# Order of record fetches, weight splits and bounds around the last token tile and the first two expert tiles

## The chip, the cores and the metric

The kernel runs on one core of one Trainium2 chip. The metric is the time on the device in microseconds (us), the median of several executions. A core has a matrix engine (TensorE, "PE" in the profile, its weight loads "PEld"), VectorE ("DVE"), ScalarE ("ACT"), GpSimd ("POOL") and a sync engine ("SP") that only issues DMAs. Each engine runs its own program in order; semaphores are the only ties between them.

## The reference

Three steps, all in float32:

1. Attention within chunks of 64 rows, 8 batches, 8 heads, 576 rows, head size 64: softmax(q k^T / 8) v. The result is reshaped to 4608 tokens of 512 values.
2. A dense layer: h = x w_in (512 to 2048), r = max(h, 0), g = s r^2 + b, x2 = g w_out (2048 to 512).
3. A mixture of 8 experts with a skip: out starts as a copy of x2. For each token with x2 . w_skip > 0, the expert e is the argmax of x2 w_gate, its weight is the softmax value of that expert, and out = x2 + weight * (max(x2 w1[e], 0) w2[e]), with w1[e] 512 x 1024 and w2[e] 1024 x 512. Other tokens keep x2.

## The kernel before, in words

Every product is made of three: each operand is split into a high part (fp32r, made by ScalarE) and a low part (the rest, made by VectorE), and lo\*hi, hi\*lo and hi\*hi are summed in PSUM. So every weight and every activation has two "split" instructions, first on ScalarE, then on VectorE, which waits for it.

**Stage 1** goes over 12 tiles of 384 tokens. Within a tile a loop over f = 0..15 (FT = 16 blocks of 128 of the 2048 columns) makes h block f + 1 (`into_h`), and adds block f to x2 (`into_x2`); ScalarE makes relu, square and the high part of g (`relu`, `hi_of_g`), VectorE the low part (`lo_of_g`). Attention for the next tile is made between them. Tile 11 is the last and has no attention beside it; its spare time on ScalarE and VectorE is used to split the weights of experts 0 and 1. These come in 8 pieces of 512 KB each (EXPERT_JOBS = 8), numbered (e,j). `jobs_at(f)` says which pieces are split in step f (of expert 0 in the odd steps from 3 on, of expert 1 from SOON_AT = 9 on, up to piece 6 of both); both engines call `split2` for them at the end of the step. The sync engine loads the next piece into a buffer when the piece before it in the same buffer has been split (`soon_done[e]`).

**Routing.** For each tile x2 is kept (`keep_x2`), multiplied by the gate, and `route_a`, `rank` (on TensorE) and `route_b` find for each token a slot in a table of records (token number, weight) in DRAM, sorted by expert. GpSimd writes the records of a tile with three scatters (`send_records`). VectorE's last steps after tile 11 count the expert tiles: the chain of small instructions L1372 to L1385 writes `bounds`, which all engines read into registers before their loops over the experts.

**Stage 2** goes over expert tiles k of 128 records, each of one expert. Tiles 0 and 1 are the first tiles of experts 0 and 1 and hold records of the first eleven token tiles only, so that they can start before tile 11 is routed; tile 2 and all later ones need all records. For tile k: the sync engine fetches 128 records into `got` (`load_records`); VectorE copies them to `idx` (`next_records`); GpSimd gathers the rows of x2 (`gather`, into `x_rows`); TensorE turns them (`turn_rows`); ScalarE and VectorE split them (`hi_of_x`, `lo_of_x`); TensorE makes h in two halves of 512 columns (`up`), ScalarE the relu (`relu2`), TensorE turns h (`turn_h`), the halves are split (`hi_of_h`, `lo_of_h`), and `down` makes y, which `finish` weighs and adds to the row; a scatter writes it to out. In TensorE's program for tile k (`expert_tile`) the order is: turn h half 0 of k, up half 1 of k, turn the rows of k + 1, down with half 0 of k, turn h half 1 of k, up half 0 of k + 1, down with half 1 of k.

Between the stages TensorE turns the rows of tile 0, turns x2 of tile 11 (L875), and multiplies it by the gate (L881) from `tail_x`, which ScalarE copies out of PSUM. The sync engine's program runs there, in this order: the weight loads by `jobs_at`, the fetch of records 0 (after the jobs of f = 11) and 1, loads of expert 2's pieces 2, 0 and 3, the stores of tile 11's x2, pieces 7 and 1, pieces 4 to 6, then the wait for `bounds`, and the fetches of records 2 and on. Pieces 0 to 3 and 7 of expert 2 use the buffers in which the last pieces of experts 0 and 1 lie until they are split: buffer 0 holds (1,6), 1 holds (1,7), 2 holds (1,5), 3 holds (0,6), 7 holds (0,7).

Of the kernel before, what the change touches and what calls it, by code (L numbers as in the profile page):

```python
# [17 lines left out]
def chunked_attention_moe(nc, first_qk_rows, first_v_rows, qk, v, w_in, w_out, moe_s, moe_b, gate_rows, gate_cols_in, w1, w2, out):  # L18
# [6 lines left out]
    FT = FF // P  # L25
# [46 lines left out]
    with ctx:  # L72
# [266 lines left out]
        def raw_place(e, j):  # L339

            if soon(e):
                return raw2[((3, 7)[j % 2], j % 3)[e]]
            return raw2[j]

        def jobs_at(f):

            found = []
            if f % 2 == 1 and f >= 3:
                found.append((0, (f - 3) // 2))
            if f >= SOON_AT:  # L350
                found.append((1, f - SOON_AT))
            return found
# [17 lines left out]
        def _(sp):  # L370
# [96 lines left out]
            for j in range(3):  # L467
                load_weights(sp, 1, j)
            for f in range(3, FT - 2):
                for e, j in jobs_at(f):  # L470
                    sp.wait_ge(soon_done[e], j + 1)
                    load_weights(sp, e, j + (2, 3)[e])
                if f == FT - 5:
                    sp.wait_ge(records_out, 16 * SUB * (TILES - 1))
                    load_records(0, 0)
            load_records(1, REGION)
            for e, n in ((1, 2), (1, 0), (0, 3)):
                last = max(j for j in range(EXPERT_JOBS - 1) if raw_place(e, j) is raw2[n])
                sp.wait_ge(soon_done[e], last + 1)
                load_weights(sp, SOON, n)  # L480
            store_rows(TILES - 1)
            for e, n in ((0, 7), (1, 1)):
                sp.wait_ge(soon_done[e], EXPERT_JOBS)
                load_weights(sp, SOON, n)
            sp.wait_ge(x2_stored, 32 * TILES)
# [8 lines left out]
            with sp.Fori(2, first_end) as t:  # L494
                load_records(t, t * P - P)
            with sp.Fori(0, second_end - first_end) as t:
                load_records(first_end + t, REGION + P + t * P)
# [413 lines left out]
        def _(act):  # L911
# [159 lines left out]

            hi_of_x(0)
            for t in range(SUB):
                act.wait_ge(tail_turned, t + 1)
                keep(tail_x[:, t, :, :], y_ps[t][:, :]).then_inc(tail_kept, 1)
            split2(0, 1, EXPERT_JOBS - 1)
            split2(1, 0, EXPERT_JOBS - 1)
            route_exp(TILES - 1)
            relu2(0, 0)
            expert_tile(0, 0, 1, False, False)  # L1080
            expert_tile(1, 1, 0, False, False)
# [20 lines left out]
        def _(dve):  # L1102
# [141 lines left out]
            def tile(i, z, attend, route):  # L1244
                for f in range(FT):
# [27 lines left out]
                    for e, j in jobs_at(f) if not attend else ():  # L1273
                        split2(e, 1 - e, j)
                    if not attend and f == FT - 2:
                        dve.wait_ge(got_in, 16)
                        dve.tensor_copy(idx[:, :], got[:, :]).then_inc(rows_held, 16)
# [83 lines left out]
            dve.tensor_copy(sent[:, :], held[:, :]).then_inc(y_ready, 32)  # L1361
            split2(0, 1, EXPERT_JOBS - 1)
            dve.wait_ge(tail_done, 1)
            dve.tensor_copy(logits[:, :, :].rearrange("p t e -> p (t e)"), logits_ps).then_inc(dots_done, DOTS)
            route_a(TILES - 1)
            route_b(TILES - 1)

            def step(n, ins):
# [16 lines left out]
            dve.tensor_copy(bounds[:, :], bounds_f[:, :]).then_inc(bounds_ready, 1)  # L1385
            lo_of_h(0, 0)
            lo_of_x(1)
            stage_rows(1)
            lo_of_h(0, 1)
            split2(1, 0, EXPERT_JOBS - 1)  # L1390
            dve.wait_ge(next_ready, 1)
            next_records(2)
            finish(0)
            take_rows(1)
# [77 lines left out]
```

## Time and profile before

| | us |
|---|---|
| median of 3 runs | 1361.82 |
| lowest, highest | 1359.89, 1362.25 |
| the profiled execution | 1362.1 |
| its span, first to last instruction | 1360.3 |
| TensorE busy | 1327.8 (98%) |
| VectorE busy | 925.6 (68%) |
| ScalarE busy | 752.6 (55%) |
| GpSimd busy | 310.3 (23%) |
| mean granted clock of TensorE | 0.994 |

How to read the rows further down. Times are us from the start of the span. A row of a timeline has the start, the duration, the engine, the line of the kernel, the operation, output <- inputs, their shapes, how often it is repeated, and in brackets how long the engine was idle before it and what ended that. A row of the windows has the stretch and its length, then busy time and number of instructions of TensorE, its weight loads, VectorE, ScalarE and GpSimd, then TensorE's granted clock as a share of 2.4 GHz, the busy share of the DMA engines, and GB/s. A row of waits has who waited, for whom, the total in us, how many times, and the longest. "to landing" is the time from the issue of a DMA to its completion, as minimum, median and maximum over the DMAs of the view. In the chain of waits each row is a step of the chain: start, length, what.

### The profile page before, as it was taken

To read this page: it belongs to the slowest core of one execution; us is meant where nothing else is said; L and a number is where in the kernel's file an instruction comes from. 1 tells how busy PE (TensorE), PEld (TensorE's weight loads), DVE (VectorE), ACT (ScalarE), POOL (GpSimd) and SP (SyncE) were. 2 spreads that over 40 slices of the span, in tenths; PEclk is the share of its full clock that TensorE was granted. 3 is DMA by queue.
4 is the path that set the end of the run, shared out by engine and by line. 5 is a ranking of instruction groups with operands and counts; after the bars stand their busy time and mean duration, and the time that the engine had idled before them with its cause. 6 is when DMAs were issued, how large, how long until landed. Compare 5 with 4: busy or idle time off the path is not lost.

```text
span 1360.3 us, 22394 instructions
## 1 busy us (share of the span) xinstructions
PE 1327.8 (98%) x7066; PEld 1169.1 (86%) x7067; DVE 925.6 (68%) x2141; ACT 752.6 (55%) x1838; POOL 310.3 (23%) x274
## 2 busy tenths in 40 slices
PE   8999999999999999999999999999898999999998
PEld 7998989899998999899998999988676778888886
DVE  4877879687886978778786878876538673333332
ACT  4886757476665656566575666646337552222221
POOL 5542222121213222221322222101111111111111
PEclk9999999999999999999999999999999999999999
DMA  7431203031221303021120302045518641111110
GB/s 276 163 121 44 98 28 108 16 100 35 72 65 34 105 21 105 25 78 59 43 94 25 102 24 101 13 155 143 189 38 293 229 156 46 39 46 39 46 38 27
DMA packets 61589, 116.95 MB, mean 86 GB/s; under 512 B 11848, under 2 KB 20296, under 8 KB 61360
## 3 DMA queue, kind: packets, MB, share of 16 engines
q1 hardware_dynamic: 44496, 81.11, 18.1%
q10 hardware_dynamic: 10880, 20.97, 4.3%
q0 software_dynamic: 6112, 13.56, 3.0%
q8 instruction: 58, 0.95, 0.3%
q14 instruction: 43, 0.35, 0.1%
HBM read 91.28 MB, written 27.08 MB: 87 GB/s over the span
## 4 chain that ended last, share of the span: by engine, by line
PE 89%; DVE 4%; issue 3%; DMA 2%; SPq 1%; DVEq 1%; ACT 1%; POOLq 0%; ACTq 0%
PE h_ps L720 30%; PE y_ps L735 28%; PE y_ps L845 10%; PE h_ps L831 10%; PE s_ps L685 3%; PE av_ps L701 3%; DVE weights_lo L1171 2%; PE t_ps L692 1%; PE t_ps L817 1%; PE s_ps L839 1%; PE av_ps L839 1%; DMA first_raw<-in_first_qk 1%; DMA wide<-x_rows,idx 1%; DVE rows_t_lo L1304 0%; DVE wide L1337 0%
## 5 line engine op out<-in xcount | busy, mean ns | idle before, releaser
L1198 DVE CUSTOM_DVE_ANT_0 products<-scratch,wide 128x512 f32<-128x512 f32 x297 | 285.6, 962 | 6.7
L720 PE MATMUL h_ps<-rows_t_hi,weights_lo 128*128 128x384 f32 (+2 forms) x776 | 262.3, 338 | 8.0 <-issue 5.8
L720 PE MATMUL h_ps<-rows_t_hi,weights_hi 128*128 128x384 f32 (+2 forms) x776 | 261.3, 337 | 0.0
L720 PE MATMUL h_ps<-rows_t_lo,weights_hi 128*128 128x384 f32 (+2 forms) x776 | 260.0, 335 | 0.0
L982 ACT ACTIVATE scratch<-h_ps 128x384 f32<-128x384 f32 x192 | 94.4, 492 | 297.0 <-PE h_ps L720 294.9
L735 PE MATMUL y_ps<-weights_hi,g_lo 128*128 128x512 f32 x576 | 229.3, 398 | 1.5 <-DVE g_lo L1177 1.5
L735 PE MATMUL y_ps<-weights_lo,g_hi 128*128 128x512 f32 x576 | 227.4, 395 | 0.0
L735 PE MATMUL y_ps<-weights_hi,g_hi 128*128 128x512 f32 x576 | 226.7, 393 | 0.0
L1177 DVE TENSOR_TENSOR g_lo<-scratch,g_hi 128x384 fp32r<-128x384 f32 x192 | 119.9, 625 | 92.1 <-ACT g_hi L913 89.5
L720 PEld LDWEIGHTS h_ps<-rows_t_hi,weights_lo 128*128 128x128 f32 x776 | 145.9, 188 | 21.7 <-issue 7.5
L541 POOL TENSOR_TENSOR qk_lo<-qk_raw,qk_hi 128x768 fp32r<-128x768 f32 x66 | 124.7, 1890 | 144.8 <-ACT qk_hi L913 144.8
L720 PEld LDWEIGHTS h_ps<-rows_t_lo,weights_hi 128*128 128x128 f32 x776 | 145.9, 188 | 7.0
L547 POOL TENSOR_TENSOR v_lo<-v_raw,v_hi 128x256 fp32r<-128x256 f32 x66 | 49.1, 745 | 436.9 <-ACT v_hi L913 436.9
L720 PEld LDWEIGHTS h_ps<-rows_t_hi,weights_hi 128*128 128x128 f32 x776 | 145.8, 188 | 0.0
L735 PEld LDWEIGHTS y_ps<-weights_hi,g_hi 128*128 128x128 f32 x576 | 108.7, 189 | 24.0
L735 PEld LDWEIGHTS y_ps<-weights_hi,g_lo 128*128 128x128 f32 x576 | 108.9, 189 | 20.7 <-DVE g_lo L1177 2.8
L735 PEld LDWEIGHTS y_ps<-weights_lo,g_hi 128*128 128x128 f32 x576 | 108.9, 189 | 17.1 <-issue 0.2
L930 ACT ACTIVATE soft<-s_ps,row_bias 64x64 f32<-64x64 f32 x528 | 120.2, 303 | 3.0
L913 ACT ACTIVATE rows_t_hi<-av_ps 64x256 fp32r<-64x256 f32 (+2 forms) x165 | 67.9, 412 | 69.9 <-PE av_ps L839 64.3
L913 ACT ACTIVATE g_hi<-scratch 128x384 fp32r<-128x384 f32 x192 | 100.8, 525 | 6.1
L845 PE MATMUL y_ps<-weights_hi,rows_t_lo 128*128 128x512 f32 x240 | 97.7, 407 | 6.5 <-DVE rows_t_lo L1304 5.5
L986 ACT ACTIVATE scratch<-scratch 128x384 f32<-128x384 f32 x192 | 99.7, 519 | 3.5
(178 smaller groups left out, 2366.3 us busy)
## 6 DMA issues: line engine op xcount, KB each, us to landing
qk_raw<-in_qk SPq DMA_DIRECT2D x66, 384.0 KB, 2.9
expert_raw<-in_w ACTq DMA_DIRECT2D x25, 512.0 KB, 5.1
expert_raw<-in_w SPq DMA_DIRECT2D x21, 512.0 KB, 5.3
out<-scratch SPq DMA_DIRECT2D x12, 768.0 KB, 4.2
x_rows<-scratch SPq DMA_DIRECT2D x12, 768.0 KB, 6.0
v_raw<-in_v SPq DMA_DIRECT2D x66, 128.0 KB, 2.0
scratch<-in_w ACTq DMA_DIRECT2D x15, 512.0 KB, 5.9
wide<-in_w_out SPq DMA_DIRECT2D x7, 512.0 KB, 4.4
```

The source lines that it names most:

```text
L541: pool.tensor_tensor(qk_rest[:, :], qk_raw[:, c % SLOTS, :], qk_top[:, :].bitcast(F32), ALU.subtract).then_inc(qk_split, 1)
L547: pool.tensor_tensor(v_lo[:, :], v_raw[:, :], v_hi[:, :].bitcast(F32), ALU.subtract).then_inc(v_split, 1)
L720: mm = pe.matmul(h_ps[f % 2][:, begin:end], w[:, f // PAIR, kt, fs], x[:, z, kt, begin:end], start=kt == 0 and n == 0, stop=kt == KT - 1 a ...
L735: mm = pe.matmul(y_ps[t][:, :], g[:, f % 2, ts], w[:, f, :], start=f == 0 and n == 0, stop=f == FT - 1 and n == 2)
L831: mm = pe.matmul(h_ps[f][:, :], x[:, kt, :], w[par][:, f, kt, :], start=kt == 0 and n == 0, stop=kt == KT - 1 and n == 2)
L845: mm = pe.matmul(y_ps[0][:, :], h[:, t, :], w[par][:, t, :], start=t == 0 and n == 0, stop=t == ET - 1 and n == 2)
L913: return act.activation(out_, in_, ACT.Copy)
L930: last = act.activation(probs[xs, c % 2, h, :], s_blocks[xs, h, x, :], ACT.Exp, bias=row_bias[xs, h:h + 1], scale=SCALE)
L982: act.activation(r_buf[f % 2], h_ps[f % 2][:, 0:TOK], ACT.Relu).then_inc(r_done, 1)
L986: act.activation(u_buf[f % 2], r_buf[f % 2], ACT.Square).then_inc(u_done, 1)
L1177: dve.tensor_tensor(GL[:, f % 2, :], u_buf[f % 2], GH[:, f % 2, :].bitcast(F32), ALU.subtract).then_inc(g_ready, 1)
L1198: dve.tensor_tensor_reduce(products[:, :], x2_sb[:, t, :], gate_w[:, e, :], 1.0, 0.0, ALU.mult, ALU.add, logits[:, t, e:e + 1]).then_inc(d ...
```

## The change

No computation is added or removed; seven places in the programs of the sync engine, ScalarE and VectorE change their order.

- `jobs_at` no longer gives jobs for f = 15; pieces (0,6) and (1,6) are split after the tail tile.
- The sync engine waits for tile 10's scatters and fetches record set 0 ahead of the jobs of f = 10 instead of after those of f = 11; VectorE copies it to `idx` at the end of f = 12 instead of f = 14.
- The sync engine loads expert 2's piece 2, stores tile 11, loads pieces 3 and 7, then 4 to 6. Pieces 0 and 1 are loaded only after the fetch of the records of tile 2 (the loop from 2 to `first_end`, which has one pass in this trace).
- ScalarE splits (0,6) after turning tile 0's rows and ahead of copying `tail_x`, (0,7) after these copies, (1,6) after `hi_of_x(1)`, and (1,7) after `hi_of_h(0,1)`.
- VectorE splits (0,6) ahead of the wait for the logits, (0,7) between `route_a` and `route_b`, (1,6) after `stage_rows(1)`, and (1,7) after `next_records(2)`.
- VectorE's `lo_of_h(0, 0)` goes ahead of the bounds.

```diff
--- before.py
+++ after.py
@@ -345,9 +345,9 @@
         def jobs_at(f):
 
             found = []
-            if f % 2 == 1 and f >= 3:
+            if f % 2 == 1 and 3 <= f < FT - 1:
                 found.append((0, (f - 3) // 2))
-            if f >= SOON_AT:
+            if SOON_AT <= f < FT - 1:
                 found.append((1, f - SOON_AT))
             return found
 
@@ -467,21 +467,20 @@
             for j in range(3):
                 load_weights(sp, 1, j)
             for f in range(3, FT - 2):
+                if f == FT - 6:
+                    sp.wait_ge(records_out, 16 * SUB * (TILES - 1))
+                    load_records(0, 0)
                 for e, j in jobs_at(f):
                     sp.wait_ge(soon_done[e], j + 1)
                     load_weights(sp, e, j + (2, 3)[e])
-                if f == FT - 5:
-                    sp.wait_ge(records_out, 16 * SUB * (TILES - 1))
-                    load_records(0, 0)
             load_records(1, REGION)
-            for e, n in ((1, 2), (1, 0), (0, 3)):
-                last = max(j for j in range(EXPERT_JOBS - 1) if raw_place(e, j) is raw2[n])
-                sp.wait_ge(soon_done[e], last + 1)
-                load_weights(sp, SOON, n)
+            sp.wait_ge(soon_done[1], EXPERT_JOBS - 2)
+            load_weights(sp, SOON, 2)
             store_rows(TILES - 1)
-            for e, n in ((0, 7), (1, 1)):
-                sp.wait_ge(soon_done[e], EXPERT_JOBS)
-                load_weights(sp, SOON, n)
+            sp.wait_ge(soon_done[0], EXPERT_JOBS - 1)
+            load_weights(sp, SOON, 3)
+            sp.wait_ge(soon_done[0], EXPERT_JOBS)
+            load_weights(sp, SOON, 7)
             sp.wait_ge(x2_stored, 32 * TILES)
             sp.wait_ge(tail_done, 1)
             for j in range(4, EXPERT_JOBS - 1):
@@ -493,6 +492,10 @@
             sp.wait_ge(records_out, 16 * SUB * TILES)
             with sp.Fori(2, first_end) as t:
                 load_records(t, t * P - P)
+            sp.wait_ge(soon_done[1], EXPERT_JOBS - 1)
+            load_weights(sp, SOON, 0)
+            sp.wait_ge(soon_done[1], EXPERT_JOBS)
+            load_weights(sp, SOON, 1)
             with sp.Fori(0, second_end - first_end) as t:
                 load_records(first_end + t, REGION + P + t * P)
             with sp.Fori(2, E) as e:
@@ -1070,14 +1073,20 @@
                 load_weights(nc.scalar, e, j)
 
             hi_of_x(0)
+            split2(0, 1, EXPERT_JOBS - 2)
             for t in range(SUB):
                 act.wait_ge(tail_turned, t + 1)
                 keep(tail_x[:, t, :, :], y_ps[t][:, :]).then_inc(tail_kept, 1)
             split2(0, 1, EXPERT_JOBS - 1)
-            split2(1, 0, EXPERT_JOBS - 1)
             route_exp(TILES - 1)
             relu2(0, 0)
-            expert_tile(0, 0, 1, False, False)
+            hi_of_h(0, 0)
+            relu2(0, 1)
+            hi_of_x(1)
+            split2(1, 0, EXPERT_JOBS - 2)
+            hi_of_h(0, 1)
+            split2(1, 0, EXPERT_JOBS - 1)
+            relu2(1, 0)
             expert_tile(1, 1, 0, False, False)
             act.wait_ge(bounds_ready, 1)
 
@@ -1272,7 +1281,7 @@
                         split(EARLY + f)
                     for e, j in jobs_at(f) if not attend else ():
                         split2(e, 1 - e, j)
-                    if not attend and f == FT - 2:
+                    if not attend and f == FT - 4:
                         dve.wait_ge(got_in, 16)
                         dve.tensor_copy(idx[:, :], got[:, :]).then_inc(rows_held, 16)
 
@@ -1359,11 +1368,13 @@
             dve.wait_ge(rows_taken, 1)
             next_records(1)
             dve.tensor_copy(sent[:, :], held[:, :]).then_inc(y_ready, 32)
-            split2(0, 1, EXPERT_JOBS - 1)
+            split2(0, 1, EXPERT_JOBS - 2)
             dve.wait_ge(tail_done, 1)
             dve.tensor_copy(logits[:, :, :].rearrange("p t e -> p (t e)"), logits_ps).then_inc(dots_done, DOTS)
             route_a(TILES - 1)
+            split2(0, 1, EXPERT_JOBS - 1)
             route_b(TILES - 1)
+            lo_of_h(0, 0)
 
             def step(n, ins):
                 ins.then_inc(bounds_step, 1)
@@ -1383,13 +1394,13 @@
             step(9 + E, dve.tensor_scalar(bounds_f[:, E + 2:E + 3], bounds_f[:, E:E + 1], 16.0, 32.0, ALU.mult, ALU.add))
             step(10 + E, dve.tensor_scalar(bounds_f[:, E + 3:], bounds_f[:, 1:E + 1], -1.0, None, ALU.add))
             dve.tensor_copy(bounds[:, :], bounds_f[:, :]).then_inc(bounds_ready, 1)
-            lo_of_h(0, 0)
             lo_of_x(1)
             stage_rows(1)
+            split2(1, 0, EXPERT_JOBS - 2)
             lo_of_h(0, 1)
-            split2(1, 0, EXPERT_JOBS - 1)
             dve.wait_ge(next_ready, 1)
             next_records(2)
+            split2(1, 0, EXPERT_JOBS - 1)
             finish(0)
             take_rows(1)
             expert_tile(1, 1, 0, False)
```

## Rows read from the trace of the kernel before

**Rows 1.** Busy time by engine, granted clock and DMA, 20 us each (the windows).

```profile
980.00:1000.00 20.00, 13.46 (x58) 10.79 (x57) 4.13 (x12) 2.97 (x5) 3.08 (x3) 0.83 0.26 94
1000.00:1020.00 20.00, 19.79 (x98) 16.07 (x97) 9.60 (x21) 9.42 (x14) 3.04 (x3) 1.00 0.12 42
```

**Rows 2.** TensorE's timeline (start, duration, ..., [idle before <- releaser]), 978 to 1010 us.

```profile
982.33 0.39 PE L831 MATMUL h_ps<-weights_hi,rows_t_hi 128*128 128x512 f32 x1
989.25 1.09 PE L817 MATMUL t_ps<-ident,wide 128*128 128x128 f32 x4 [6.54 <-DMA wide<-x_rows,idx]
...
993.89 0.60 PE L839 MATMUL av_ps<-ident,wide 128*128 128x128 f32 x4
...
1003.01 0.60 PE L817 MATMUL t_ps<-ident,wide 128*128 128x128 f32 x4
...
1006.42 0.60 PE L839 MATMUL av_ps<-ident,wide 128*128 128x128 f32 x4
```

**Rows 3.** The chain of waits in order of time (start, length, what).

```profile
975.39 1.14 DVE weights_lo L1171
...
978.52 0.48 SPq L491
...
980.21 4.63 DMA got<-table
...
986.03 3.09 DMA wide<-x_rows,idx
```

**Rows 4.** The sync engine's own waits, 950 to 982 us.

```profile
SPq L364 <- DVE weights_lo L1171: 20.8, 3, 13.5
```

**Rows 5.** The three record scatters of tile 10: issue times, time to landing.

```profile
L560 POOL DMA_INDIRECT table<-record,slot x3: 972/1301/1843, 932.2 to 936.0; - x3
...
DMA to landing us min/median/max: 5.3/6.6/10.4
```

**Rows 6.** The three record scatters of tile 11: issue times, time to landing.

```profile
L560 POOL DMA_INDIRECT table<-record,slot x3: 973/992/1024, 966.9 to 969.5; - x3
...
DMA to landing us min/median/max: 3.4/3.5/3.7
```

**Rows 7.** Landing of the five expert-weight loads issued 933 to 940 us.

```profile
DMA to landing us min/median/max: 3.6/9.0/9.8
```

**Rows 8.** Landing of the four expert-weight loads issued 976 to 979 us.

```profile
DMA to landing us min/median/max: 3.7/5.4/6.7
```

**Rows 9.** Landing of the record fetches issued 940 to 1000 us.

```profile
DMA to landing us min/median/max: 1.7/2.7/4.6
```

**Rows 10.** Landing of the row gathers issued 900 to 1000 us.

```profile
DMA to landing us min/median/max: 2.5/4.0/7.0
```

**Rows 11.** ScalarE's timeline, 940 to 965 us.

```profile
945.05 1.99 ACT L913 ACTIVATE weights_hi<-expert_raw 128x1024 fp32r<-128x1024 f32 x2
947.73 0.49 ACT L982 ACTIVATE scratch<-h_ps 128x384 f32<-128x384 f32 x1 [0.68 <-PE h_ps L720]
...
958.85 1.57 ACT L913 ACTIVATE scratch<-y_ps 128x512 f32<-128x512 f32 x3
```

**Rows 12.** VectorE's timeline, 955 to 975 us.

```profile
956.78 2.06 DVE L1187 SCALAR_TENSOR_TENSOR scratch<-y_ps,s_col,bias 128x512 f32<-128x512 f32 x3
...
961.39 1.23 DVE L1171 TENSOR_TENSOR weights_lo<-expert_raw,weights_hi 128x1024 fp32r<-128x1024 f32 x1 [0.98 <-ACT weights_hi L913]
...
965.80 0.16 DVE L1240 TENSOR_TENSOR slot<-slot_f,far 128x3 int32<-128x3 f32 x1
...
969.82 0.67 DVE L1304 TENSOR_TENSOR rows_t_lo<-s_ps,rows_t_hi 128x512 fp32r<-128x512 f32 x1
```

**Rows 13.** TensorE's timeline, 955 to 975 us.

```profile
957.69 0.63 PE L817 MATMUL t_ps<-ident,wide 128*128 128x128 f32 x4 [1.17 <-DMA wide<-x_rows,idx]
...
959.58 2.82 PE L881 MATMUL s_ps<-gate_cols,scratch 128*128 128x9 f32 x24
...
970.59 0.47 PE L845 MATMUL y_ps<-weights_hi,rows_t_lo 128*128 128x512 f32 x1 [0.48 <-issue]
```

## The prediction, made before the changed kernel was run

> **What bounds the kernel now.** TensorE is busy nearly everywhere, so I looked for the stretch where it is not. The windows of 20 us come first: from 980 to 1000 us TensorE is busy for 13.46 us at a mean granted clock of 0.83, from 1000 to 1020 for 19.79 us at 1.00 [rows 1]. All that the change touches lies between 930 and 1010 us, so the second view is TensorE's timeline there. Its last product of expert tile 1's second half of h starts at 982.33; then it idles 6.54 us until the rows gathered for tile 2 have landed, at 989.25 [rows 2]. The next tile's copy of the same stretch (transposes of rows, twelve products, transposes of h) takes 1006.42 - 1003.01 = 3.41 us. The h products are spaced 0.23 us, so without the wait the transposes would start at 982.56 and the next ones at 985.97; they start at 993.89. The stall thus costs 7.92 us: 6.7 of waiting and the rest at the lower clock, since the granted clock is 0.83 on average in this window, that is, TensorE came out of its idleness at 1.2 GHz instead of 2.4 (its four transposes take 1.09 us beside 0.60 in the next tile [rows 2]).
>
> Third, the chain of waits tells what made the rows late [rows 3]: VectorE's last split of expert 1 (975.39), then the sync engine's loads, its register loads of the bounds from 978.52, the fetch of the records at 980.21, which takes 4.63 us, and the gather at 986.03, which takes 3.09. The sync engine stood 13.5 us on that split [rows 4] with load (1,1) of expert 2. Behind it in its program stood three more loads and the fetch of the records for tile 2, for which everything else was ready: the bounds were being finished when lo_of_h(0,0), the next VectorE instruction after them, began at 969.82 [rows 12], and the third scatter of tile 11's records, issued at 969.5, landed at 969.5 + 3.7 = 973.2 [rows 6]. So the fetch could have gone 7 us earlier.
>
> **Part 1, the fetch of tile 2's records (the main term).** Removed: the wait on split (1,7) ahead of the loads and of the fetch. Moved: loads 0 and 1 of expert 2 behind the fetch. I follow the new chain. Split (0,7) now sits between route_a and route_b. It costs 1.23 us on VectorE [rows 12], some 0.4 of which is won back because the logits are copied about 0.3 us earlier and nothing stands ahead of them. The slot of the records, at 965.80 before, comes at 966.63, 0.83 later, and the third scatter is issued at 970.3. lo_of_h(0,0) now stands ahead of the bounds (0.67 us, and about 0.4 of waiting for its high half), so the bounds, 969.9 before, are ready at 971.7. The sync engine's register loads take 980.21 - 978.52 = 1.7 us [rows 3], to 973.4; they do not bind, the scatter does. It lands at 973.8 to 974.0 if it takes 3.4 to 3.7 us as before [rows 6]. But four loads of 512 KB (pieces 7, 4, 5, 6), which in the kernel before are issued from 976.5 on, now go out at 965.2 to 966.7, ahead of and beside the scatters. Their old group needed up to 6.7 us each to land [rows 8], 8.2 us from first issue to last landing; from 965.2 that ends at 973.4. Bounds for the scatter: 3.4 us [rows 6], and 10.4 us, which the last scatter of tile 10 took among five such loads [rows 5, 7]. I take 4.2, nearer the quiet rows, since all four loads are out 3.6 us before this scatter, while tile 10's last had three issued after it and beside it: landed at 974.5. The fetch follows at 974.9 and lands after 1.7 us (bounds 1.7 and 4.6 [rows 9]; 4.6 was with four loads just ahead of it, now the queue is empty), at 976.7. Before, the gather started at 986.03, 1.2 us after the fetch had landed at 980.21 + 4.63 = 984.84 [rows 3], with the copy into idx between them; VectorE is free from 974.6 on, so the gather starts at 977.9. It needs 2.5 to 7.0 us [rows 10]; loads 0 and 1, 1 MB, now go out at 975.4 and 978.2 beside it, so I take 4.2, by the 4.0 of the middle row: 982.1.
>
> When does TensorE want it? Parts 2 and 3 bring it there 0.6 us earlier than 982.56, at 981.9. A wait of about 0.3 us stays, too short to lower the clock by anything seen here. Part 1: 7.92 - 0.3 = 7.6 us gained.
>
> The Trainium skill, page "DMA: Bandwidth & Descriptors", section "Queues, rings and completion order", says two things that pull apart here. Its arbitration rule lets each DMA engine take turns between queues packet by packet; by that the scatter would land in its quiet 3.5 us and the sum would be 0.3 us better. Its ordering rule says that the write which raises a semaphore lands only after every earlier write of that DMA engine, across its queues; by that rule the scatter's completion waits for the loads' data, as the 10.4 us row looks, and it speaks against putting four loads ahead of it: the sum would be as I have it or, with loads that drain slowly, that of rival A.
>
> **Part 2, what moves out of the tail (f = 15).** Splits (0,6) and (1,6) leave VectorE ahead of keep_x2. keep_x2 started at 956.78 only because two splits were in front [rows 12]; TensorE had ended its last product at 957.69 - 1.17 = 956.52 [rows 13], so the three parts can now follow the products as they end, and the last is kept some 1.4 us earlier. The 1.17 us of idleness ahead of turn_rows(0) ended with the gather of tile 0's rows [rows 13]; its records are now fetched before the loads of f = 10 and copied at f = 12, so these rows land several us earlier and this wait goes too. But what TensorE needs next is tail_x from ScalarE, whose three copies began at 958.85 [rows 11]. ScalarE now turns x at 957.2 and then has split (0,6), 1.0 us (two take 1.99 [rows 11]), ahead of these copies: they begin at 958.7. So of 1.2 us on TensorE only 0.15 reach the logits (959.58 before [rows 13]). Bounds: 0 and 1.2.
>
> **Part 3, lo_of_h(0,0) ahead of the bounds.** Before, VectorE did it at 969.82, behind the bounds, and TensorE's down products waited 0.48 us for it, to 970.59 [rows 12, 13]. It now runs at 967.5, and the wait goes: 0.48 gained. Late next is lo_of_x(1), behind the bounds: 971.7 to 972.4, wanted by first_half(1) at 973.15, so 0.7 us of cover is left; beyond it each us of bounds is a us of TensorE. Splits (1,6) and (1,7) fall into time in which VectorE had nothing to do between its split at 975.39 and the fetch's landing at 984.84 [rows 3], and (1,7), done by 978.1, is wanted only at 982.4. Expert 2's pieces 0 and 1 land by 983; ScalarE first reads them some 22 us later, so that costs nothing.
>
> **Part 4, the price in the tail tile.** At f = 10 the sync engine now waits for tile 10's scatters ahead of loads (1,4), (0,6), (1,5). The last scatter was issued at 936.0 and landed after 10.4 us, at 946.4 [rows 5], among these very loads, whose own landing took up to 9.8 us [rows 7]. With three of them held back I expect it to land at about 942 (bounds 939.4 by the quiet 3.4 us [rows 6], and 946.4). Load (1,4) goes out at 942.4 and lands by about 947 (3.7 to 5.4 us [rows 8]). ScalarE wants it at 946.0, the second of the pair at 945.05, and has 0.68 us to spare before the next relu [rows 11]; TensorE has a block of h products of about 2 us between that relu and its use. So nothing is lost until the load lands after about 948.3, that is, unless the scatter lands after 943.4. VectorE's new wait for the records, at f = 12, holds lo_of_g(13) behind it; it ends at 944 to 945, when that instruction is due anyway. I take 0.
>
> **Sum.** 7.6 + 0.15 + 0.48 = 8.2 us off the profiled execution's 1362.1 us (span 1360.3): 1353.9. That execution is 0.3 us above the median of the runs, 1361.82; I predict 1353.7 for the median.
>
> **Rivals.** A: the loads delay the records and something of the stall stays. The scatter takes 6.6 us [rows 5], to 976.9, fetch to 979.0, gather started 980.3, 4.0 us, landed 984.3: 2.4 us of wait, 1356.0. For it: rows 5 and 7. Against it: rows 8, where four loads drained in 8.2 us. B: the records of tile 10 still land at 946.4, so (1,4) lands at 946.8 + 3.7 = 950.5; ScalarE's split is 950.5 - 946.0 = 4.5 us late, 3.8 after its slack. TensorE loses between 0 and 3.8, I take the middle, 1.9: 1355.6. C: the wait changes its owner. Scatter and fetch both meet the loads at their worst, 10.4 and 4.6 us, and gather 5.0 beside loads 0 and 1: 970.3 + 10.4 + 0.4 + 4.6 + 1.2 + 5.0 = 991.9, later than 989.25 by 2.7 us, so the kernel is slower, 1364.5. It decides from the scatter's landing on: with these fetch and gather times the stall is as long as before when it takes 7.7 us, and it is longer beyond. D: the fetch lands no earlier than before because only part of this comes true (scatter 7.7 us): 1361.8 less the small gains, about 1361.
>
> **Numbers.** Forecast 0.61, A 0.17, B 0.13, C 0.04, D 0.05. The forecast's own range is 1352.4 (all 1.2 us of part 2, no wait left) to 1355.2. A and B, also together, reach to 1358, and I add 0.9 us below for the scatter of the runs: 1351.5 to 1358.2. A measurement of this kernel can tell 0.2%, 2.7 us, from no change. Forecast, A and B are faster by more; D is the same; C is at the edge. So 0.91, 0.05, 0.04.
>
> **What would show it.** Right: a fetch at about 975 us in the trace, no idleness over 1 us ahead of TensorE's transposes at 982, granted clock 1.00 from 980 to 1000, no 0.48 us ahead of the down products, and logits at about the old time. Wrong: a fetch later than 978 (A, C), ScalarE waiting for a weight load at 946 to 950 (B), TensorE waiting for lo_of_x(1), or a gather of 5 us or more.

## The result, and the profile after

The changed kernel takes 1352.53 us (median of 5 runs, 1352.33 to 1355.31) beside 1362.24 us of the kernel before: a ratio of 0.9938, 95% interval 0.9923 to 0.9954. That is 9.7 us less; the interval allows 6.3 to 10.5. The forecast was 1353.7 us, 8.2 us less than before. The two profiled executions, 1362.1 and 1355.16 us, lie 6.9 us apart: the one of the changed kernel is 2.6 us above its median.

The stall is gone. The windows of the changed kernel, beside [rows 1]:

```profile
980.00:1000.00 20.00, 20.00 (x101) 16.39 (x100) 7.10 (x18) 4.57 (x8) 3.25 (x4) 1.00 0.17 57
```

TensorE's timeline of the changed kernel answers to [rows 2, 13]; the numbers in front are start and duration:

```profile
958.41 3.79 PE L884 MATMUL s_ps<-gate_cols,scratch 128*128 128x9 f32 x24 [0.90 <-ACT scratch L916]
968.21 0.66 PE L842 MATMUL s_ps<-ident,wide 128*128 128x128 f32 x4 [0.69 <-ACT wide L1040]
971.46 0.60 PE L820 MATMUL t_ps<-ident,wide 128*128 128x128 f32 x4
974.65 0.60 PE L842 MATMUL av_ps<-ident,wide 128*128 128x128 f32 x4
983.77 0.60 PE L820 MATMUL t_ps<-ident,wide 128*128 128x128 f32 x4
986.98 0.60 PE L842 MATMUL av_ps<-ident,wide 128*128 128x128 f32 x4
```

No transposes of rows (L820) have a bracket: TensorE waits for no gather, neither at 955.60 nor at 983.77. But the logits take 3.79 us instead of 2.82, and this is the surprise of the trace. The windows of the changed kernel show why (the third column from the right is the granted clock):

```profile
955.00:960.00 5.00, 4.10 (x35) 3.71 (x33) 4.02 (x9) 3.76 (x6) 0.90 (x1) 1.00 0.51 190
960.00:966.00 6.00, 6.00 (x21) 4.84 (x20) 3.31 (x14) 0.41 (x2) 0.29 (x1) 0.50 0.72 237
```

From 960 to 966 us TensorE has work all the time and only the 1.2 GHz level of its clock. In the profiled execution of before this time was at full clock. The windows of the kernel before:

```profile
960.00:966.00 6.00, 5.57 (x43) 4.55 (x42) 4.42 (x23) 2.92 (x5) 1.00 (x1) 1.00 1.02 367
```

The sync engine's waits from 940 to 990 us, beside [rows 4]:

```profile
SPq L490 <- DVE bounds L1396: 6.4, 1, 6.4
...
SPq L493 <- DMA table<-record,slot: 0.3, 1, 0.3
```

It now waits for the bounds and then 0.3 us for the last scatter, and fetches at 975.66 what it fetched at 980.21; the copy into idx runs at 977.50:

```profile
977.50 0.17 DVE L1320 COPY idx<-got 128x2 int32<-128x2 int32 x1 [0.90 <-DMA got<-table]
```

**One measure for all traces.** Stage 1 ends anywhere within some 6 us from one execution to the next. So I compare a *stretch* within each trace: from the first product of the last tail block (it has the bracket "DVE g_lo") to the h transposes of tile 1 (av_ps, the second one). It begins here in TensorE's timelines, before and changed:

```profile
954.16 0.50 PE L735 MATMUL y_ps<-weights_hi,g_lo 128*128 128x512 f32 x1 [0.20 <-DVE g_lo L1177]
```

```profile
953.41 0.50 PE L738 MATMUL y_ps<-weights_hi,g_lo 128*128 128x512 f32 x1 [0.20 <-DVE g_lo L1186]
```

Before: 954.16 to 993.89, 39.73 us. Changed: 953.41 to 986.98, 33.57 us. What is left after it, 1360.3 - 993.89 and 1353.4 - 986.98, is 366.4 us in both. Ahead of it, the tail tile from its first x2 block (f = 0) to its last (f = 15) takes 61.8 us in all fourteen traces (61.77 to 61.85), with the change and without. What differs is the start of that tile, from 889.1 to 894.7 us, and no instruction ahead of it was changed. So in the traces all of the change's effect lies in the stretch. ScalarE's timeline of the changed kernel has the relu of [rows 11] with the same 0.68 us to spare:

```profile
946.98 0.49 ACT L985 ACTIVATE scratch<-h_ps 128x384 f32<-128x384 f32 x1 [0.68 <-PE h_ps L723]
```

Its 6.16 us come apart like this. The stall: by the changed kernel's own undisturbed tile (986.98 - 983.77 = 3.21 us) it had cost 993.89 - 982.56 - 3.21 = 8.12 us. From the last block to the logits 5.42 became 5.00: 0.42. From turn_rows(1) to the next transposes, 973.43 - 969.51 = 3.92 before [rows 13 hold the wait in it], 3.19 now: 0.73. The logits and the products after them, up to the h transposes (959.58 to 966.25 before, 6.67 us), take 968.21 - 958.41 = 9.80 us: 3.13 lost to the clock. Sum: 8.12 + 0.42 + 0.73 - 3.13 = 6.14. The medians differ by 9.7 us, 3.5 more than the stretch; no trace shows where, since the executions at the median were not profiled.

### The profile page after: what moved, and what is told of

Same layout as the page of the kernel before. It is cut to its first block, busy times and chain, and to the rows that moved or that the text cites. A ratio compares the mean times of both kernels' runs of the same rounds, so it can differ in the third digit from the quotient of the medians.

```text
span 1353.4 us, 22395 instructions
## 1 busy us (share of the span) xinstructions
PE 1329.0 (98%) x7066; PEld 1171.8 (87%) x7067; DVE 927.9 (69%) x2141; ACT 753.0 (56%) x1838; POOL 311.1 (23%) x274
## 4 chain that ended last, share of the span: by engine, by line
PE 90%; DVE 5%; issue 3%; ACT 1%; DVEq 1%; POOLq 0%; POOL 0%; ACTq 0%
PE h_ps L723 29%; PE y_ps L738 28%; PE y_ps L848 10%; PE h_ps L834 10%; PE s_ps L688 3%; PE av_ps L704 3%; DVE weights_lo L1180 2%; PE t_ps L695 1%; PE s_ps L842 1%; PE t_ps L820 1%; PE av_ps L842 1%; PE h_ps L651 0%; DVE rows_t_lo L1313 0%; DVE weights_lo L1171 0%; DVE g_lo L1186 0%
## 5 line engine op out<-in xcount | busy, mean ns | idle before, releaser
L834 PE MATMUL h_ps<-weights_hi,rows_t_lo 128*128 128x512 f32 x244 | 102.1, 418 | 0.0
```

The costliest lines, as they stand in the source:

```text
L834: mm = pe.matmul(h_ps[f][:, :], x[:, kt, :], w[par][:, f, kt, :], start=kt == 0 and n == 0, stop=kt == KT - 1 and n == 2)
```

## The experiments

The kernels ran in groups, each group on one chip with the kernel before beside it, whose medians were 1363.20 us (e1 to e4), 1363.06 (e5, e7, e8, e9), 1366.17 (e6, e10, e11) and 1362.66 (e12). Between groups the ratio and the stretch can be compared, the bare times cannot. The ratios of the kernels other than e2 and e10 have intervals that overlap: the runs' times alone separate none of them, and what follows rests on the traces, one of each kernel.

| kernel | median us | ratio, 95% | stretch us | low clock in 955 to 970 | wait for gather 2 |
|---|---|---|---|---|---|
| before | 1362.24 | | 39.73 | none | 6.54 |
| changed | 1352.53 | 0.9938 (0.9923 to 0.9954) | 33.57 | long | none |
| e9, changed again | 1353.11 | 0.9928 (0.9912 to 0.9944) | 33.55 | long | none |
| e11, changed again | 1356.93 (one run) | | 33.56 | long | none |
| e1, fetch only | 1354.01 | 0.9932 (0.9915 to 0.9950) | 33.11 | none | 1.69 |
| e2, fetch back | 1362.62 | 1.0001 (0.9980 to 1.0021) | 42.18 | long | 6.89 |
| e3, tail_x first | 1352.45 | 0.9931 (0.9904 to 0.9958) | 31.26 | none | 1.58 |
| e4, bounds first | 1354.26 | 0.9936 (0.9918 to 0.9955) | 32.11 | short | none |
| e5, gap filled | 1353.26 | 0.9928 (0.9913 to 0.9944) | 31.94 | short | none |
| e6, records 0 back | 1357.92 | 0.9930 (0.9913 to 0.9947) | 32.93 | short | none |
| e7, loads behind fetch | 1357.05 | 0.9950 (0.9933 to 0.9966) | 34.40 | none | 2.18 |
| e8, three edits | 1352.87 | 0.9937 (0.9915 to 0.9960) | 31.37 | none | 1.67 |
| e10, loads behind gather | 1363.41 | 0.9979 (0.9955 to 1.0003) | 31.08 | short | none |
| e12, next fetch first | 1350.53 | 0.9926 (0.9899 to 0.9953) | 29.52 | none | none |

"Long" is about 6.8 us at 1.2 GHz, "short" about 3.4 us. From the logits to the h transposes of tile 0 it then takes 9.8 or 8.2 us instead of 6.7.

**e1: the fetch alone, put into the kernel before.**

```diff
-            for e, n in ((0, 7), (1, 1)):
-                sp.wait_ge(soon_done[e], EXPERT_JOBS)
-                load_weights(sp, SOON, n)
+            sp.wait_ge(soon_done[0], EXPERT_JOBS)
+            load_weights(sp, SOON, 7)
...
                 load_records(t, t * P - P)
+            sp.wait_ge(soon_done[1], EXPERT_JOBS)
+            load_weights(sp, SOON, 1)
```

> The kernel before with one edit: the load of expert 2's piece 1, with its wait on split (1,7), stands behind the fetch of tile 2's records. Theory T1 (the changed kernel's gain is nearly all the stall ahead of tile 2's rows): the 6.5 us of idleness ahead of the transposes at 982 go, and with them the half clock after it: 7.5 to 7.9 us faster than before, about 0.9943. Rival R1 (the stall is only a symptom: with the fetch early, the gather would still be late for another reason, and most of the changed kernel's gain comes from the tail and the bounds): less than 3 us faster.

Measured: ratio 0.9932 (9.2 us); the stretch is 6.6 us shorter. T1 stands and R1 falls: this one move gives, within the noise, as much as the whole change. A wait of 1.69 us stays, where I had expected none. TensorE's timeline and the chain of waits of e1:

```profile
983.54 0.63 PE L818 MATMUL t_ps<-ident,wide 128*128 128x128 f32 x4 [1.69 <-DMA wide<-x_rows,idx]
```

```profile
968.75 8.15 DMA table<-record,slot
...
977.25 1.72 DMA got<-table
...
980.16 3.24 DMA wide<-x_rows,idx
```

The last scatter took 8.15 us, not the 3.7 of [rows 6]: the loads of pieces 4 to 6 were issued just ahead of it, the last one at 968.24.

**e2: the fetch put back, in the changed kernel.**

```diff
             load_weights(sp, SOON, 7)
+            sp.wait_ge(soon_done[1], EXPERT_JOBS)
+            load_weights(sp, SOON, 1)
             sp.wait_ge(x2_stored, 32 * TILES)
...
             dve.wait_ge(next_ready, 1)
-            next_records(2)
-            split2(1, 0, EXPERT_JOBS - 1)
```

(On VectorE the split stands ahead of this wait, and the load behind the fetch is gone.)

> The changed kernel with the load of expert 2's piece 1 ahead of tile 2's fetch again, and so split (1,7) ahead of the copy of these records on VectorE. T1: the stall of 6 to 8 us comes back, 0.6 to 2.5 us of the gain over before stay (lo_of_h ahead of the bounds and the tail). R1: most of the gain stays.

TensorE's timeline of e2:

```profile
988.56 1.08 PE L820 MATMUL t_ps<-ident,wide 128*128 128x128 f32 x4 [6.89 <-DMA wide<-x_rows,idx]
```

T1 stands: the stall is back, with the slow transposes behind it. The expected 0.6 to 2.5 us of gain don't show in the median (ratio 1.0001), but the interval, 0.9980 to 1.0021, does not rule them out. The profiled execution had the long low clock as well, and its stretch is 2.45 us longer than before's: there the clock took 3.1 us, more than the tail and the bounds gave (0.42 + 0.73).

**e3: ScalarE copies tail_x ahead of split (0,6).**

```diff
-            split2(0, 1, EXPERT_JOBS - 2)
             for t in range(SUB):
                 act.wait_ge(tail_turned, t + 1)
                 keep(tail_x[:, t, :, :], y_ps[t][:, :]).then_inc(tail_kept, 1)
+            split2(0, 1, EXPERT_JOBS - 2)
```

> The changed kernel, but ScalarE copies tail_x first and makes split (0,6) after it. My part 2 says that this split on ScalarE eats 1.0 of the 1.2 us that TensorE could have in the tail: the idle 0.9 us ahead of the logits go, and the kernel is 0.9 to 1.1 us faster than the changed one where the clock is the same. Theory T2 (the half clock of 960 to 967 us in the profiled execution of the changed kernel, worth about 3 us, comes after this low activity and appears in some executions only): with the idleness gone, fewer executions show it or none, and the median may gain up to 3 us more. Rival R2 (the dip has nothing to do with this gap): the same two levels of time, 2.8 us apart, about 1 us lower both.

TensorE's timeline of e3:

```profile
957.71 2.82 PE L884 MATMUL s_ps<-gate_cols,scratch 128*128 128x9 f32 x24
...
981.73 0.63 PE L820 MATMUL t_ps<-ident,wide 128*128 128x128 f32 x4 [1.58 <-DMA wide<-x_rows,idx]
```

From the last block (953.69) to the logits it takes 4.02 us instead of 5.00: the 0.98 us that I had put on that split. The clock stays full, and then a wait of 1.58 us appears, behind a scatter of 5.55 us and a gather of 4.02. The chain of waits of e3:

```profile
968.75 5.55 DMA table<-record,slot
...
977.57 4.02 DMA wide<-x_rows,idx
```

The time is hardly lower than the changed kernel's: its median lies inside that one's runs. So neither the expected 0.9 to 1.1 us nor more can be told from the times.

**e4: lo_of_h(0,0) behind the bounds again.**

```diff
             route_b(TILES - 1)
-            lo_of_h(0, 0)
...
+            lo_of_h(0, 0)
             lo_of_x(1)
```

> The changed kernel, but lo_of_h(0,0) behind the bounds as before. My part 3: the down products wait again, and now longer than the 0.48 us of before, since the bounds start 0.8 us later: 0.5 to 1.3 us slower than the changed kernel. Rival: the bounds are ready 1 us sooner and the records with them, and the time is the same, which would mean that a wait for the gather is left in the changed kernel.

Measured: 1354.26 us, 1.1 to 1.7 above the changed kernel's two medians, with ratios that overlap. In the trace the down products lose only 0.17 us (969.03 to 972.39, 3.36 us, beside 3.19), perhaps because the short low clock had made TensorE late anyway. In line with part 3, but not shown by it. The rival fails: the bounds come sooner, but the fetch of tile 2's records does not, 21.00 us into the stretch beside 21.10 in e5, which also has the short low clock: the sync engine waits 3.0 us for the last scatter instead of 0.6.

**e9 and e11: the changed kernel again; e5: the gap filled.** The edit of e5, ahead of the logits:

```diff
+            weights_by(0, EXPERT_JOBS // 4)
+            for _ in range(4):
+                pe.matmul(h_ps[1][:, :], WH[1][:, 0:P], WH[1][:, 0:512], start=True, stop=True)
             pe.wait_ge(cols_in, 16)
```

> The changed kernel unaltered, on the same chip as the next three, to compare them with it and to see a second profiled execution. In the first one the granted clock was 0.50 from 960 to 966.6 us and nothing waited for the gather of tile 2. Theory T3: in an execution without that low clock TensorE reaches the transposes of tile 2's rows about 3 us sooner and then waits 0.5 to 2.5 us for the gather, as in the two experiments at full clock (1.6 and 1.7 us), so that both kinds of execution take nearly the same time. Rival R3: without the low clock there is no wait either, and such an execution is 3 us faster than the first profile, measured from the last tail block to the h transposes of tile 1 (33.6 us there).

> The changed kernel with four products of weights (128x512, result unused) put into TensorE's idle 0.9 us ahead of the logits. T2 (the low clock from 960 on follows the idleness and the small products of 956 to 960 us): the granted clock stays at 1.00 from 955 to 970, and in exchange the wait for the gather shows, 1 to 2.5 us: time equal to the changed kernel within 1.5 us. R2 (the low clock is unrelated to that gap): 0.50 in the same place.

> The changed kernel once more, one profile, in the hope of an execution at full clock from 955 to 970. T3: if so, a wait of 0.5 to 2.5 us for the gather of tile 2; R3: none.

Both further profiles of the changed kernel had the long low clock and a stretch of 33.55 and 33.56 us, so T3 could not be seen directly. The runs' times say little. Leaving out e11's one run, of the eleven timed executions of the changed kernel, the five whose mean clock was 0.999 or more took 1351.15 to 1353.64 (median 1352.44), the six at 0.997 or less 1352.53 to 1356.18 (median 1354.23). That is 1.8 us, not 3.1, but taken by groups the difference is 2.8 us in the first and 0.4 in e9's, and nothing tells where in these runs the clock was low.

e5 says more, since it is the changed kernel but for four products. Its gather of tile 2's rows was issued at 976.00 and landed after 4.09 us, at 980.09; TensorE took the rows at 980.72, with 0.63 us to spare, and the short low clock had cost it 8.2 - 6.7 = 1.5 us. An estimate from these numbers: at full clock, with the records no earlier, it would have waited some 0.9 us. T3 is likely, not shown.

e5 speaks against T2: without any idleness of TensorE from 952 to 961 us the clock still fell, though for the short time. Its time equals e9's within 0.2 us. Its windows:

```profile
955.00:960.00 5.00, 5.00 (x40) 4.49 (x39) 2.68 (x8) 3.73 (x6) 1.19 (x1) 1.00 0.81 295
960.00:965.00 5.00, 4.47 (x21) 2.96 (x19) 4.19 (x20) 0.71 (x2) 0.00 (x0) 0.66 0.68 209
```

Over all profiles, the clock fell in six of the seven with the 0.9 us gap ahead of the logits (changed, e9, e11, e2, e4, e6, but not e7) and in two of the seven without it (e5, e10; not in before, e1, e3, e8, e12). The gap neither suffices nor is it needed, and fourteen profiles are too few to show that it matters at all; what decides stays open.

**e6: records 0 fetched and copied late again.**

```diff
-                if f == FT - 6:
-                    sp.wait_ge(records_out, 16 * SUB * (TILES - 1))
-                    load_records(0, 0)
                 for e, j in jobs_at(f):
...
+                if f == FT - 5:
+                    sp.wait_ge(records_out, 16 * SUB * (TILES - 1))
+                    load_records(0, 0)
...
-                    if not attend and f == FT - 4:
+                    if not attend and f == FT - 2:
```

> The changed kernel with the fetch of records 0 after the jobs of f = 11 and their copy at f = 14, as before. My part 2: the rows of tile 0 land late again, TensorE waits for them 0.5 to 1.2 us ahead of turn_rows(0), but what it needs next is tail_x, so the time stays within 0.5 us or is up to 0.9 us longer. My part 4: the last scatter of tile 10 takes 8 to 10.4 us again among the loads; in the changed kernel the sync engine's wait for it ended at 940.3, about 4 us after its issue. Rival: slower by over 1.5 us, which would mean that the early fetch is a large part of the gain.

TensorE's timeline of e6:

```profile
959.43 0.63 PE L820 MATMUL t_ps<-ident,wide 128*128 128x128 f32 x4 [0.77 <-DMA wide<-x_rows,idx]
...
962.27 2.82 PE L884 MATMUL s_ps<-gate_cols,scratch 128*128 128x9 f32 x24 [0.91 <-ACT scratch L916]
```

The wait of 0.77 us is back, and the logits begin 5.93 us after the last block instead of 5.00. So the early fetch is worth 0.9 us there, the upper end of what was expected, since the 0.95 us of ScalarE's split come on top of the wait. The ratio, 0.9930, is the changed kernel's, so the rival's 1.5 us don't show. Its last scatter of tile 10, issued at 938.1, let the fetch go at 948.35, after some 10 us as in [rows 5]; in the changed kernel the issue is at 935.2 and the fetch at 940.33, 5.1 us:

```profile
940.33 0.34 SPq L461 DMA_DIRECT2D got<-table  x1
```

**e7 and e8: the four loads behind the fetch.** e7 moves pieces 7, 4, 5, 6 behind the fetch of tile 2's records; e8 is e7 with e3's edit and `split2(0, 1, EXPERT_JOBS - 1)` of VectorE behind `route_b`.

```diff
             load_weights(sp, SOON, 3)
-            sp.wait_ge(soon_done[0], EXPERT_JOBS)
-            load_weights(sp, SOON, 7)
-            sp.wait_ge(x2_stored, 32 * TILES)
-            sp.wait_ge(tail_done, 1)
-            for j in range(4, EXPERT_JOBS - 1):
-                load_weights(sp, SOON, j)
...
                 load_records(t, t * P - P)
+            sp.wait_ge(soon_done[0], EXPERT_JOBS)
+            load_weights(sp, SOON, 7)
+            sp.wait_ge(x2_stored, 32 * TILES)
+            sp.wait_ge(tail_done, 1)
+            for j in range(4, EXPERT_JOBS - 1):
+                load_weights(sp, SOON, j)
```

> The changed kernel, but the loads of expert 2's pieces 7, 4, 5 and 6 stand behind the fetch of tile 2's records. Theory T4 (these four loads delay the last scatter of tile 11's records, which took 5.6 and 8.2 us in the experiments at full clock, 3.7 in the kernel before): the last scatter lands 3.4 to 3.8 us after its issue, the fetch 2 to 4 us sooner than with the loads ahead of it, and the wait for the gather is gone: up to 1.7 us faster than the changed kernel in executions at full clock, equal in the others. Rival R4 (the scatter's landing is late for another reason): 5 us or more, and no gain. Price to look for: the gather now has six loads beside it, up to 7 us.

> The changed kernel with three edits: ScalarE copies tail_x ahead of split (0,6); the four loads stand behind the fetch; VectorE makes split (0,7) behind route_b, so that the slots of the records are ready 1.2 us sooner. If T2 to T4 hold, there is neither low clock nor a wait for the gather: 31.3 us less 1.6 = 29.7 us from the last tail block to the h transposes of tile 1, 2 to 3 us faster than the changed kernel. If the gather among six loads takes up to 7 us, the wait stays and the gain is 1 us.

The chain of waits of e7:

```profile
969.25 3.79 DMA table<-record,slot
...
973.39 1.74 DMA got<-table
...
976.32 6.39 DMA wide<-x_rows,idx
```

and of e8:

```profile
967.36 3.89 DMA table<-record,slot
...
974.53 6.40 DMA wide<-x_rows,idx
```

T4 is right about the scatter: 3.79 and 3.89 us instead of 5.55 and 8.15. But the price that was to be looked for came in full: the gather beside the loads takes 6.4 us, and the wait stays (2.18 and 1.67 us). e7's median is 3.9 us above that of the changed kernel on the same chip (e9), with intervals of the ratios that overlap (0.9933 to 0.9966 and 0.9912 to 0.9944). In its trace the transposes behind the wait take 0.85 us instead of 0.60, the granted clock from 980 to 1000 us is 0.91 on average, and the stretch is 34.40 us. TensorE's timeline of e7:

```profile
982.85 0.85 PE L820 MATMUL t_ps<-ident,wide 128*128 128x128 f32 x4 [2.18 <-DMA wide<-x_rows,idx]
```

e8, where 1 us of gain was expected in this case, has none that shows: 1352.87 us beside 1353.11.

With the loads ahead of the scatter, its time goes with how soon behind the last of them it is issued:

| | issued behind the last load, us | the scatter took, us | landed after that load's issue, us |
|---|---|---|---|
| e1 | 0.5 | 8.15 | 8.7 |
| e3 | 3.3 | 5.55 | 8.9 |
| e5 | 3.6 | 4.7 | 8.4 |
| e9, the changed kernel | 4.1 | 4.1 | 8.3 |

It lands 8.3 to 8.9 us after that load's issue, whenever it is issued itself. In these four it is thus the loads that set when the fetch can go, and an earlier scatter alone would have gained little.

**e10 and e12: no load beside any step of the chain.** e10 is e8 with `sp.wait_ge(rows_in, 48)` ahead of the six loads. e12 puts the next fetch ahead of them too:

```diff
+            load_records(first_end, REGION + P)
             sp.wait_ge(rows_in, 48)
...
-            with sp.Fori(0, second_end - first_end) as t:
+            with sp.If(second_end > first_end + 1):
+                with sp.Fori(1, second_end - first_end) as t:
```

> The last experiment's kernel (tail_x first, split (0,7) behind route_b, four loads behind the fetch) with one more wait: the sync engine waits until the gather of tile 2's rows has landed before it issues the six loads. Theory T5 (whatever of the records' chain runs beside 512 KB loads is slow: 5.6 to 8.2 us instead of 3.8 for the scatter, 4.0 to 6.4 us instead of 3.1 for the gather): the gather lands in 3.1 to 3.5 us, TensorE does not wait for it, and from the last tail block to the h transposes of tile 1 it takes 29.6 to 29.9 us beside 31.4; about 1351 us, 1.5 to 2 us faster than the changed kernel. Rival R5 (the gather is slow for its position, not for the loads, or the loads, all later by 10 us, collide with the next gather or the splits of expert 2): a wait of over 1 us stays, or comes back at tile 3 or at 1005 us.

> The kernel of the experiment with the loads behind the gather, but the fetch of tile 3's records stands ahead of the six loads (in the last one it stood behind them and took 9.0 us). T5: the scatter lands in 3.8 to 4.0 us, the gather of tile 2 in 3.1 to 3.4 us, the next fetch in 1.7 us, and TensorE waits for none of them: 29.5 us at full clock (31 with a short low clock) from the last tail block to the h transposes of tile 1, beside 33.1 to 33.6 in the changed kernel and the fetch-only experiment; 9.5 to 11.5 us faster than before on the same chip, ratio 0.9915 to 0.993. Rival R5: the six loads, now at 983, delay the fetch of tile 4 or its gather, and a wait of 1 us or more comes at tile 3 or 4: no faster than the changed kernel (0.9928 to 0.9938).

The chain of waits of e10:

```profile
972.25 4.00 DMA table<-record,slot
...
979.53 3.36 DMA wide<-x_rows,idx
...
986.58 9.01 DMA got<-table
```

Scatter and gather are quick, as T5 has it, and nothing waits at tile 2. The stretch, 31.08 us, has the short low clock in it; less the 1.6 us that this cost (8.3 - 6.7) it is 29.5, about as expected. But the fetch of tile 3's records is now the one behind 3 MB of loads, and it comes 6 us or more later in the stretch than in e7 and e8, where it took 8.8 and 8.2 us without TensorE waiting. VectorE waits 9.0 us for it with lo_of_h behind that wait, and TensorE stands 5.63 us:

```profile
996.53 0.79 PE L849 MATMUL y_ps<-weights_hi,rows_t_lo 128*128 128x512 f32 x1 [5.63 <-DVE rows_t_lo L1314]
```

So the stretch is short and the kernel hardly better than before (0.9979, interval 0.9955 to 1.0003). R5 had named this tile, though for the gather and not for the fetch. e12 mends just that. TensorE's timeline of e12:

```profile
974.93 0.60 PE L845 MATMUL s_ps<-ident,wide 128*128 128x128 f32 x4
978.14 0.60 PE L823 MATMUL t_ps<-ident,wide 128*128 128x128 f32 x4
981.34 0.60 PE L845 MATMUL av_ps<-ident,wide 128*128 128x128 f32 x4
```

From 951.82 it is 29.52 us, where 29.5 was expected, with no wait and full clock. e12 has the lowest median of all, 1350.53 us, 12.1 below its own before. Against the changed kernel's profiles the stretch is 4.0 us shorter, but 3.1 of it is their low clock, which e12's other runs may have as well. The fair comparison is e8, at full clock too: 31.37 us, 1.85 more, of which the wait was 1.67. The collision has moved on once more, as R5 had it: the gather of tile 3, issued at 981.72 beside the six loads, took 6.2 us. But TensorE does not wait for it. The ratios, 0.9926 (0.9899 to 0.9953) and 0.9928 or 0.9938, can't tell e12 and the changed kernel apart; one run of e12 took 1361.53.

## Why the prediction was right

- **The total.** 8.2 us forecast, 9.7 between the medians, 6.9 between the profiled executions, 6.2 in the stretch. The mechanism was right; that the number came within 1.5 us is in part luck. The low clock, which the forecast did not have, took 3.1 us of the stretch, and the medians show 3.5 us more than the stretch, which no trace accounts for. (1361.82 - 8.2 is 1353.6, not 1353.7; that is rounding.)
- **The bound.** Right: the stall ahead of tile 2's rows, made by the sync engine's place in its queue. e1 and e2, one part done and one undone, show it. Forecast 7.6 us, in the stretch 8.1.
- **Part 1's chain, step by step.** Scatter issue expected at 970.3, was 970.9; the scatter to take 4.2 us, and the sync engine's wait for it ended about 4.4 after the issue; fetch 974.9, was 975.66; its landing expected at 976.7, and the copy behind it came at 977.5; gather 977.9, was 978.6. As this stretch began 0.75 us earlier than before's, scatter, fetch and gather are 1.4 to 1.5 us late within it; 0.97 of that are the logits at the low clock. TensorE, expected to wait 0.3 us, waited not at all, but the low clock had made it 3.1 us late; by e5, some 0.9 us of wait would be likely without it. "They do not bind, the scatter does" was right by little: the register loads of the bounds came just 0.3 us ahead of the scatter.
- **Rival A**, loads beside the records' chain, has a real mechanism, and I gave it 0.17 as an alternative. Its size did not come in the changed kernel: the scatter took 4.1 us in e9, not 6.6. But e1 and e3, at full clock, wait 1.7 and 1.6 us behind a slow scatter, e7 and e8 2.2 and 1.7 behind a slow gather. The Trainium skill, page "DMA: Bandwidth & Descriptors", section "Queues, rings and completion order", has the ordering rule (a completion lands only after earlier writes of its DMA engine, across queues), and the traces fit it: 5.6 and 8.2 us beside loads, 3.8 to 4.0 without. But no run here separates it from a plain sharing of the DMA engines; in e5 the first of the three scatters, issued 1.0 us behind the last load, landed at 970.9, 0.8 us ahead of it.
- **Part 2.** The step that was off is "So of 1.2 us on TensorE only 0.15 reach the logits": 0.42 did, and ScalarE's split holds another 0.98 (e3). Mis-sized by 0.3 us: ScalarE's copies began 4.4 us into the stretch, 4.7 before.
- **Part 3.** 0.48 forecast, 0.73 in the trace; e4, which took it back, lost 0.17 and couldn't confirm it.
- **Part 4.** Taken at 0, and it was 0: the scatter of tile 10 landed by 940.3 (942 expected, 943.4 the limit), and the relu at 946.98 had the same 0.68 us to spare as in [rows 11]. The tail tile took 61.8 us as before. So rival B did not come; e6 with its 10 us shows what the loads had done to the scatter.
- **C and D** did not come: the scatter took neither 7.7 nor 10.4 us in the changed kernel. Missing altogether: the low clock from 960 to 966.6. It costs TensorE 3.1 us and the kernel probably less, as part of that would have been a wait for the gather.

## What to carry to other kernels

A small transfer on a critical chain (here 1 KB of records) should be looked at twice: for what stands ahead of it in the queue of the engine that issues it, and for which bulk loads are in flight when it goes out. Moving the loads away from one step puts them beside the next; hold them until the last step of the chain has landed, and send the next tile's small fetch ahead of them. In e12 that took the waits out of the trace; a gain in time over the changed kernel is not shown. And when a stall is removed, compare traces over a stretch that begins and ends on the same instructions: here the tail tile began up to 5.6 us apart from one profiled execution to the next, with the same code ahead of it.

## What the runs showed of the hardware

- The same 128-row scatter of records (the last of three) took 3.7 to 4.0 us with no 512 KB load in flight (e7, e8, e10) or one issued 6.9 us ahead of it (before), 4.1 to 8.2 behind three or four of them (e9, e5, e3, e1), and 10 among five (before's tile 10); the same gather 3.1 to 3.4 without (before, e10, e12), 4.0 beside two (e3, e5) and 6.4 beside six (e7, e8); a 1 KB fetch 1.7, and 8.2 to 9.0 right behind six loads on its own queue (e8, e7, e10).
- TensorE's clock fell to 1.2 GHz while it was fully busy, in eight of fourteen profiles, behind transposes and products only 9 columns wide (the logits). It fell 1.5 to 1.9 us after the first of these products and stayed low for about 6.8 us in four (changed, e9, e11, e2), or fell 2.1 to 3.9 us after it, for about 3.4 us (e4, e5, e6, e10); in e4, e5 and e6 the products 9 columns wide had ended 0.7 to 1.1 us before. It fell in six of the seven with a gap of 0.9 us among them and in two of the seven without, too few to show that the gap matters. In e5, one of these two, four filler products took the gap's place.
